# Fused attention and two gated layers on one core: x loaded by head sides, upper parts of W_out on ScalarE, layer-2 operand sums on GpSimd

## What is computed

```python
# attention: batch 4, 8 heads, 576 tokens, head size 64, block-causal mask
scores = scale * q @ k.T ; softmax ; attn @ v
# x: (2304 tokens, 512), heads side by side
h = x @ w_in                     # 512 -> 2048
g = h * clip(h + 3, 0, 6) / 6
x2 = g @ w_out                   # 2048 -> 512
h = x2 @ w2_in
g = h * tanh(softplus(h))
out = g @ w2_out
```

## Time and profile before

| What | Value |
|---|---|
| median of 3 runs | 977.72 us (974.49 to 978.66) |
| the profiled execution's own time | 975.95 us |
| its span | 974.0 us |
| PE busy | 952.0 us, 98% of the span |
| DVE, ACT, POOL busy | 746.6, 643.6, 431.3 us |
| mean granted clock of PE | 0.998 |

### The profile page before, as it was taken

The page is one execution under the profiler, slowest core; times in us unless marked ns, Lnnn a source line. Parts: engine busy times, 40 slices in busy tenths (PEclk is TensorE's granted clock), DMA queues, the critical chain, the costliest instruction groups (busy, mean ns, idle before and its releaser), DMA issues.

```text
span 974.0 us, 17754 instructions
## 1 busy us (share of the span) xinstructions
PE 952.0 (98%) x6028; PEld 848.0 (87%) x6028; DVE 746.6 (77%) x1417; ACT 643.6 (66%) x1431; POOL 431.3 (44%) x410
## 2 busy tenths in 40 slices
PE   8999999999999999999899999999999999999998
PEld 7898888999887888888788988998998988988896
DVE  7898898774868686789788787777887777777654
ACT  7999999754544445454445557777777777776663
POOL 7899779665837596776867670000000000000000
PEclk9999999999999999999999999999999999999999
DMA  7988898657698978788786546555655654565255
GB/s 217 270 240 243 258 273 234 173 153 238 220 291 291 290 256 252 234 294 252 269 275 212 209 170 217 176 202 195 215 197 184 231 210 155 182 248 187 90 193 194
DMA packets 84601, 216.42 MB, mean 222 GB/s; under 512 B 10144, under 2 KB 16928, under 8 KB 84512
## 3 DMA queue, kind: packets, MB, share of 16 engines
q1 hardware_dynamic: 84368, 215.01, 67.6%
q10 hardware_dynamic: 144, 0.29, 0.1%
HBM read 162.07 MB, written 39.92 MB: 207 GB/s over the span
## 4 chain that ended last, share of the span: by engine, by line
PE 67%; DVE 7%; DMA 6%; SPq 4%; POOL 3%; issue 2%; ACT 1%; ACTq 0%; DVEq 0%; POOLq 0%
PE psum L1021 32%; PE psum L904 10%; PE psum L906 10%; PE psum L905 10%; DMA ext_d<-ext_made 3%; PE psum L849 2%; PE psum L828 2%; DVE ebuf L1624 1%; PE psum L808 1%; POOL osplit L1885 1%; SPq L646 1%; DVE glo L1630 1%; PE psum L809 1%; SPq L648 1%; DVE ext_made L1530 1%
## 5 line engine op out<-in xcount | busy, mean ns | idle before, releaser
L1021 PE MATMUL psum<-ghi,osplit 128*128 128x512 f32 (+1 forms) x640 | 216.7, 372 | 2.1 <-POOL osplit L1885 2.1
L904 PE MATMUL psum<-xhi,whi 128*128 128x256 f32 (+1 forms) x640 | 188.0, 294 | 5.1 <-ACT snap L1242 2.5
L906 PE MATMUL psum<-xhi,wlo 128*128 128x256 f32 (+1 forms) x640 | 187.2, 293 | 0.0
L905 PE MATMUL psum<-xlo,whi 128*128 128x256 f32 (+1 forms) x640 | 187.0, 292 | 0.0
L1021 PE MATMUL psum<-osplit,ghi 128*128 128x512 f32 x576 | 180.7, 395 | 1.3 <-DVE glo L1630 1.3
L1630 DVE SCALAR_TENSOR_TENSOR glo<-ebuf,ghi 128x512 fp32r<-128x512 f32 x144 | 126.5, 878 | 22.9 <-ACT ghi L1290 14.8
L904 PEld LDWEIGHTS psum<-xhi,whi 128*128 128x128 f32 x640 | 121.1, 189 | 19.0 <-ACT snap L1242 4.4
L1290 ACT ACTIVATE ghi<-ebuf 128x512 fp32r<-128x512 f32 x144 | 90.4, 628 | 66.9 <-DVE ebuf L1624 46.2
L1021 PEld LDWEIGHTS psum<-ghi,osplit 128*128 128x128 f32 x640 | 118.5, 190 | 18.4 <-issue 2.7
L1885 POOL TENSOR_TENSOR osplit<-oraw,osplit 128x512 fp32r<-128x512 f32 x80 | 117.2, 1468 | 38.1 <-ACT osplit L1209 34.0
L905 PEld LDWEIGHTS psum<-xlo,whi 128*128 128x128 f32 x640 | 121.2, 189 | 10.5
(11 more groups left out here) (120 smaller groups left out, 2147.4 us busy)
## 6 DMA issues: line engine op xcount, KB each, us to landing
ext<-ext_d SPq DMA_DIRECT2D x56, 768.0 KB, 4.4
osplit<-o_d SPq DMA_DIRECT2D x80, 512.0 KB, 5.3
oraw<-in_w_out SPq DMA_DIRECT2D x80, 256.0 KB, 5.8
wraw<-in_w_in SPq DMA_DIRECT2D x26, 512.0 KB, 6.0
ext_d<-ext_made SPq DMA_DIRECT2D x32, 384.0 KB, 6.2
attn_t<-ostage SPq DMA_DIRECT2D x32, 288.0 KB, 3.7
qkin<-in_qk SPq DMA_DIRECT2D x30, 288.0 KB, 3.7
kparts<-kparts SPq DMA_DIRECT2D x30, 288.0 KB, 4.2
```

Source lines behind the costliest of these rows:

```text
L904: pe.matmul(dst, hi, xh, start=(start and cc == 0), stop=False, skip_group_check=True)
L905: pe.matmul(dst, hi, xl, start=False, stop=False, skip_group_check=True)
L906: last = pe.matmul(dst, lo, xh, start=False, stop=(stop and cc == 1), skip_group_check=True)
L1021: last = pe.matmul(bank(Y_BANK + c, n), stat, mov, start=(first and m == 0), stop=(final and m == 2), skip_group_check=True)
```

## The change

1. The x load of blocks 1 to 4 is made by sides in place of chunks (`load_x_side`): for side h two DMAs of the heads' summands (L656 of the new kernel) and one that spreads two rows of inverse sums (L660), so 6 DMAs for a half in place of 8, with the same bytes. For blocks 2 to 4 side 0 is issued near the head of SP's step, ahead of `load_ext`, and side 1 where the whole load stood.
2. W_out's hi parts of tiles 32 to 79 go from POOL to ACT (`first_os`, bound SPLIT_OS in place of ACT_OS).
3. The three sums for each pair of the second layer's extra operands go from DVE (`mix_w`) to POOL (`mix_late`), with a semaphore of their own, `late_mixed`.
4. On POOL in step 0 the sums of block 1's second half (`mix_x(1, 1)`) come one W_out tile later.

```diff
--- before.py
+++ after.py
@@ -118,7 +118,6 @@
 TILES = [(layer_of(g), t) for g in range(STEPS) for t in tiles_of(g)]
 TILE0 = [sum(len(tiles_of(k)) for k in range(g)) for g in range(STEPS + 1)]
 FIRST_OS = OR
-ACT_OS = TILE0[FIRST_STEP[2]]
 SPLIT_OS = TILE0[LAYER]
...
@@ -173,8 +172,8 @@
 X_SPLITS = per_block((3, 6, 8))
 X_MIXES = per_block((1, 2, 8))
 X_LOADS = [[sum(16 * n(b) for b in range(blk)) for blk in range(NBLK + 1)] for n in (
-    lambda b: (16 if KIND[b] == SHORT else 8) if b < NBL else 1,
-    lambda b: 0 if KIND[b] == SHORT else 8 if b < NBL else 2 if b > NBL else 1)]
+    lambda b: (16 if KIND[b] == SHORT else 6) if b < NBL else 1,
+    lambda b: 0 if KIND[b] == SHORT else 6 if b < NBL else 2 if b > NBL else 1)]

 JOBS = ([(0, p, True, False) for p in range(PAIRS)] + [(0, p, False, True) for p in range(PAIRS)] +
...
@@ -185,7 +184,7 @@
 NEARLY, HALVED = len(EARLY_JOBS), 6
 EARLY_LOADS = {0: (0, 0), 1: (0, 1), 2: (1, 0), 3: (1, 1), 6: (2, 0), 7: (2, 1), 9: (3, 0), 10: (3, 1),
                19: (4, 0), 20: (4, 1), 21: (5, 0), 22: (5, 1)}
-EARLY_X_LOAD, NEXT_X_LOAD = tuple(range(11, 19)), (27, 28, 29, 30)
+EARLY_X_LOAD, NEXT_X_LOAD = tuple(range(11, 19)), (27, 29)
 EARLY_X_ADD, EARLY_X_MIX = (19, 20, 21, 22), 23
 EARLY_X_HI, EARLY_X_LO = (23, 24, 25), (24, 25, 26)
 EARLY_O_LOAD = (23, 24, 25)
...
@@ -226,7 +225,8 @@

-MIXED = [sum(3 if e else 1 for _, _, _, e in JOBS[NEARLY:m]) for m in range(len(JOBS) + 1)]
+MIXED = [sum(0 if layer == 1 and e else 3 if e else 1 for layer, _, _, e in JOBS[NEARLY:m])
+         for m in range(len(JOBS) + 1)]

 def own(m):
...
@@ -649,7 +650,17 @@
                                  r_d[2 * c + h:2 * c + h + 1, cols].to_broadcast([DH, cols.stop - cols.start])
                                  ).then_inc(done, 16)
-            def load_x(blk, cc):
+            def load_x_side(x, cc, h, cols, done):
+                rows = slice(h * DH, (h + 1) * DH)
+                for i in range(2):
+                    sp.dma_start(x[rows, i, 0:2, :],
+                                 attn_t[4 * i + 2 * cc + h, :, cols].rearrange("(s d) t -> d s t", s=2)
+                                 ).then_inc(done, 16)
+                rinvs = r_d[2 * cc + h:HEADS:4, cols]
+                sp.dma_start(x[rows, :, 2, :], rinvs.unsqueeze(0).broadcast_to([DH, 2, cols.stop - cols.start])
+                             ).then_inc(done, 16)
+
+            def load_x(blk, cc, sides=range(2)):
                 t0 = first_token(blk)
                 cols = slice(t0, t0 + width(blk))
                 if blk >= LATE_X:
...
@@ -658,8 +669,8 @@
                     sp.wait_ge(x_lo, x_index(blk, cc, 0))
                 if blk < NBL:
                     attention_stored(-(-cols.stop // SEQ))
-                    for i in range(2):
-                        load_x_chunk(x_staged(blk, cc, i), 2 * i + cc, cols, x_loaded[cc])
+                    for h in sides:
+                        load_x_side(xst_late if blk == 1 and cc == 1 else xst, cc, h, cols, x_loaded[cc])
                     return
                 covered = sum(1 for b in range(NBL) if first_token(b) < cols.stop)
                 for c in range(DC):
...
@@ -676,14 +687,17 @@
                     for i in range(2):
                         sp.dma_start(x_staged(blk, 1, i)[:, 0, :], rows[1, :, i, :]).then_inc(x_loaded[1], 16)
-            def next_x(s):
+            def next_x(s, side):
                 for blk in range(2, LATE_X):
                     t = s - (FIRST_STEP[blk] - 2)
-                    if t == -8:
-                        load_x(blk, 0)
-                    if t == -4 and KIND[blk] == QUAD:
-                        load_x(blk, 1)
+                    sides = (side,) if blk < NBL else range(2 * side)
+                    if t == -8 and sides:
+                        load_x(blk, 0, sides)
+                    if t == -4 and sides and KIND[blk] == QUAD:
+                        load_x(blk, 1, sides)
+                if side == 0:
+                    return
                 for blk, t in late_blocks(s):
                     if t in LATE_LOAD and (LATE_LOAD[t] == 0 or KIND[blk] == QUAD):
                         load_x(blk, LATE_LOAD[t])
...
@@ -729,11 +743,10 @@
                 if n in EARLY_O_LOAD:
                     load_o(EARLY_O_LOAD.index(n))
                 if n in NEXT_X_LOAD:
-                    i, side = divmod(NEXT_X_LOAD.index(n), 2)
-                    if i == 0 and side == 0:
+                    if n == NEXT_X_LOAD[0]:
                         sp.wait_ge(x_lo, X_SPLITS[1])
                         attention_stored(2)
-                    load_x_chunk(x_staged(1, 0, i), 2 * i, slice(HT, HT + TB), x_loaded[0], (side,))
+                    load_x_side(xst, 0, NEXT_X_LOAD.index(n), slice(HT, HT + TB), x_loaded[0])
                 if in_use(n) and n != LAST:
                     store_o(n)
                 if in_use(n) and n != LAST and n % HEADS == HEADS - 1:
...
@@ -752,6 +765,7 @@
                         store_ext_hi(m)
                 for t in ahead_at(s - 1):
                     store_ahead_hi(t)
+                next_x(s, 0)
                 if quad(s + 3):
                     load_ext(s + 3)
                 if first_of_block(s):
...
@@ -776,7 +790,7 @@
                     stream_o(i)
                 for i in raw_at(s)[1:2]:
                     load_o(i)
-                next_x(s)
+                next_x(s, 1)
                 for i in raw_at(s)[2:]:
                     load_o(i)
                 for i in streams[2:]:
...
@@ -1157,7 +1171,10 @@
             def split_ext_hi(m):
                 layer, p, _, _ = JOBS[m]
-                act.wait_ge(w_mixed, MIXED[m + 1])
+                if layer == 0:
+                    act.wait_ge(w_mixed, MIXED[m + 1])
+                else:
+                    act.wait_ge(late_mixed, 3 * (p + 1))
                 act.wait_ge(ext_hi_stored, 16 * (layer * PAIRS + p))
                 nc.scalar.activation(ext_made[:, 0:EXT], wraw[m % 2][:, A_COLS:RES], ACT.Copy).then_inc(w_hi, 1)
...
@@ -1313,7 +1330,7 @@
             def first_os(s, k):
-                todo = [i for i in splits_at(s) if i < ACT_OS]
+                todo = [i for i in splits_at(s) if i < SPLIT_OS]
                 for i in todo[k:k + 1]:
                     split_o_hi(i)
...
@@ -1532,7 +1549,8 @@
             def mixing_jobs(s):
                 for m in jobs_at(s)[0:1]:
-                    mix_w(m)
+                    if JOBS[m][0] == 0 or JOBS[m][2]:
+                        mix_w(m)
             def resident_jobs(s):
                 for k, m in enumerate(jobs_at(s)):
...
@@ -1816,6 +1834,17 @@
                     add_x(1, 2)
                     scale_x(1, 2)
+            def mix_late(m):
+
+                p, raw = JOBS[m][1], wraw[m % 2]
+                a11, a12, a22, a21 = (raw[:, k * A_COLS:(k + 1) * A_COLS] for k in range(4))
+                pool.wait_ge(w_loaded[m % 2], w_level(m))
+                nc.gpsimd.tensor_tensor(a21, a11, a21, ALU.subtract).then_inc(late_mixed, 1)
+                pool.wait_ge(late_mixed, 3 * p + 1)
+                nc.gpsimd.tensor_tensor(a22, a22, a21, ALU.subtract).then_inc(late_mixed, 1)
+                pool.wait_ge(late_mixed, 3 * p + 2)
+                nc.gpsimd.tensor_tensor(a12, a12, a22, ALU.subtract).then_inc(late_mixed, 1)
+
             def split_early_hi(m):
                 pool.wait_ge(early_mixed, m + 1)
...
@@ -1874,12 +1903,12 @@
             def split_o(i):
                 o, raw = osplit[i % OS2], oraw[i % OR]
-                if i < FIRST_OS or i >= ACT_OS:
+                if i < FIRST_OS:
                     pool.wait_ge(o_loaded[i % OR], 16 * (i // OR + 1))
                     if i >= OS2:
                         pool.wait_ge(y_step, y_tile(i - OS2))
                     nc.gpsimd.tensor_copy(o[:, 0:D], raw[:, :]).then_inc(o_hi, 1)
-                    pool.wait_ge(o_hi, i + 1 if i < FIRST_OS else i + 1 - (ACT_OS - FIRST_OS))
+                    pool.wait_ge(o_hi, i + 1)
                 else:
                     pool.wait_ge(first_o_hi, i + 1 - FIRST_OS)
                 nc.gpsimd.tensor_tensor(o[:, D:2 * D], raw[:, :], o[:, 0:D].bitcast(F32), ALU.subtract
...
@@ -1925,10 +1954,14 @@
                 if s == 0:
                     add_x(1, 3)
                     scale_x(1, 3)
-                    mix_x(1, 1)
+                for m in jobs_at(s):
+                    if JOBS[m][0] == 1 and JOBS[m][3]:
+                        mix_late(m)
                 next_x(s, 0)
                 for i in todo[1:2]:
                     split_o(i)
+                if s == 0:
+                    mix_x(1, 1)
                 next_x(s, 1)
                 for i in todo[2:]:
                     split_o(i)
```

More of the change, by code:

```diff
@@ L368, in build @@
         w_mixed = sem("w_mixed")
+        late_mixed = sem("late_mixed")
         w_hi = sem("w_hi")
```

## The result

The change is slower. Nine runs of each kernel gave 982.80 us (978.05 to 986.65) against 976.68 us (974.12 to 979.12): a ratio of 1.0064, with a 95% interval of 1.0046 to 1.0082. The forecast was 971.6 us, in a range of 967.0 to 976.5. The profiled execution has a span of 981.6 us, against 974.0 before.

A forecast was written before the change was run, and what follows sets the result against it. It took PE's idle waits and a half-clock stretch, at most 11.7 us, as recoverable. Gains of 2.9 + 1.0 + 0.3 + 1.9 = 6.1 us took 975.95 to 969.85, plus 1.77 for the runs' median: 971.6 us, range 967.0 to 976.5.

The forecast's parts named there:

- the lo store's: Steps 19 to 26: the extra operands' lo store lands some 2 us earlier, so 0.5 us of PE's 2.32 us wait stay.
- steps 19 to 26: 425 to 500 us: sums moved to POOL remove 5.4 us of PE's waits, 3.5 are spent again, 1.9 us gained.
- the five short waits: PE's waits from 425 to 500 us other than the 2.32 us one: 3.1 us, from DVE's sums, all to go.
- Steps 0 and 1: Near 213 us: mix_x(1, 1) later on POOL ends PE's 2.10 us wait and half clock, 0.9 stay: 2.9 us gained.
- Blocks 2 and 3: Hi parts on ACT end the 402 us wait, 1.0 us; x by sides eases the 317 us wait, 0.3 us.
- The 0.3 us of the lo store's chain: PE's 1.46 us wait at 317 us, ending DVE's chain behind a lo store: 0.3 us gained, ends -1 and 1.46.
- Step 26: POOL's work on block 4's second x half ends late, so PE waits 2.5 us at step 26; ends 0 and 5.
- The 27.5: POOL's time in us from x's landing to its last lo part, with five casts gone and six sums added.
- Rival 4: ACT stands behind W_out's loads, 2 us lost in each of nine steps: slower, 989.6 us; chance 0.08.
- Rival 3: The shared SBUF port gives DVE's time back: 974.5 us, or 976.2 with the clock falling; sign POOL sums over 1.2; chance 0.12.
- Rival 2: POOL sets block 4's start, PE waits 5 us at step 26: 974.1 us; sign x landing after 18 us; chance 0.16.
- The slower case: Slower by over 0.5%: given only to ACT standing behind W_out's loads, 989.6 us; chance 0.08.

The follow-up runs named there:

- side0_late_step22: The change with side 0 of the x load moved back behind the lo store and second W_out tile in step 22 alone: ratio 1.0023 to the kernel before.
- before_again: The kernel before, unchanged, profiled once more; no ratio is given, and its wait of PE for tile 4 was 1.00 us.
- six_dmas: hi_on_act_alone with the x load by sides in six DMAs, all at the old place: ratio 0.9978 to the kernel before.
- side0_late: The change with side 0 of each x load of blocks 2 to 4 back just ahead of side 1: ratio 0.9998 to the kernel before.
- hi_on_pool: The change with the hi parts of W_out's tiles 32 to 79 back on POOL: ratio 1.0127 to the kernel before.
- hi_on_act_alone: The kernel before with only the hi parts of W_out's tiles 32 to 79 moved to ACT: ratio 0.9971 to the kernel before.

## Why the prediction was wrong

- **The failed step** is the lo store's, in the part on steps 19 to 26. The text saw all of it: "The store one step before now stands behind side 0's three DMAs on SP's queue, as do `ext`, the weights and a W_out tile, and side 0 waits at the step's head for POOL's lo parts of the first half. DVE without its sums has room for that." It put no price on that wait. The runs put about 4 us on it (`side0_late_step22` against the change) and show why the room didn't help: the chain runs through the single buffer of the lo part, and a DVE that waits for a store has no use for room. The price could have been bounded from rows of before: POOL's lo parts of the first half ended at 446.55, and three sums a step at 0.8 to 1.19 us, less two casts of 0.91, in three steps make them 1.8 to 5.3 us later, while the early place asks for them 3.6 us earlier (446.46 against 450.08). That is an estimate of 1.9 to 5.4 us of waiting for SP; the trace has 4.2.
- **What the sums' move did win:** the five short waits (3.1 us) that were to go from 425 to 500 us went but for one of 0.40 us. The long ones took their place.
- **Steps 0 and 1, 2.9 us:** nothing that the runs show (0.9992 alone). The signs were there (under 1 us, clock at full), but for another reason: the wait for tile 4 didn't go. It is 0.89 us in the change and 1.00 in `before_again`, and ACT's hi part sets it, not `mix_x`. The size was read from one execution in which `mix_x` took 1 us longer, the wait was twice its usual length and the clock fell.
- **Blocks 2 and 3, 1.0 + 0.3 us:** right in direction, and the hi parts on ACT were worth more than forecast, 2.8 us (0.7 to 5.1). The 0.3 us of the lo store's chain didn't show: PE's wait there was 1.46 us in before, 1.63 in `before_again` and 1.85 in the change. The early side 0 took some 2 us back: in step 2 its DMAs go ahead of two W_out tiles, ACT waited 2.78, 2.37 and 1.21 us for tiles where before waited 2.33 and 0.29, and PE 1.97 at 251. All five kernels with side 0 early in step 2 have a wait of 1.6 to 2.0 us there; of those without, one has 1.16 (`six_dmas`) and the others 0.3 or none. The prediction had "the bytes queued are the same", which is true and says nothing about which of them is needed first.
- **Step 26, 2.5 us:** the wait was forecast at 2.5 and measured at 2.41, and 2.40 in `side0_late`. That the number agrees in the change is luck: POOL's chain from its first work on x took 31.6 us, not 27.5, and x landed 19.7 us after step 22's start (457.34 + 9.6 against 447.26 on ACT), not 17.1, but PE had been delayed as much by its other waits. The 27.5 is also a slip: 27.4 - 4.5 + 4.8 is 27.7.
- **The rivals.** Rival 4's mechanism isn't it: ACT waited once for `oraw` after 425 us, 3.24 us, and PE didn't wait for that; `hi_on_pool` is slower yet. Rival 3: POOL's sums took 0.75 to 1.08 us on the mean, under the 1.2 that was its sign; DVE's lo parts of g were as long as before (1.17 us against 1.18), and DVE's instructions from 425 to 500 us took 49.89 / 61 = 0.82 us on the mean as 65.80 / 80 = 0.82 before. The Trainium skill's rule in page "SBUF — State Buffer", section "Who interferes with whom" (a DVE instruction with two SBUF inputs contends with a GpSimd one that reads SBUF), made no extra loss that this mean shows. Rival 2 held in part: x landed later than its sign of 18 us, but PE's wait at step 26 was 2.41 us and not 5. The slower case should have been the one with SP's queue, and had no chance of its own.
- The Trainium skill, page "DMA: Bandwidth & Descriptors", section "Anatomy of one DMA — SWDGE (gpsimd) path", says that a semaphore wait of a DMA happens on the sequencer that issues it, not in the DMA engines. The trace agrees: SP's queue stood 4.2 us for side 0 alone, and the lo store behind it, ready from 448.15 us, went out at 454.56.

## What to carry to other kernels

A DMA that waits for a semaphore is a barrier for everything behind it in its issuing queue: before moving one earlier, list what is behind it and compare the moment when the queue arrives there with the moment when its condition comes true, on the slowest engine's timeline and after the other parts of the change. Two moves that cost nothing alone can meet in one wait, so ask of each pair whether one makes the other's condition late. And a term that rests on one wait of one execution needs a second profile, above all where a fall of the clock hangs on it.

## Unexpected in the hardware

- The clock doesn't fall after every wait of the same length: it stayed at 2.4 GHz after 2.32 us and after the 2.41 us at 470 us in `hi_on_act_alone`, and fell for a few us after 2.10, 1.97 and 2.41 us in the profiles shown above. At one and the same place the 1.97 us at 251 in the change were followed by 0.59 from 252 to 256 us, and the 1.98 us at 251 in `side0_late_step22` by 1.00 from 250 to 256. A wait of 2 us is worth 2 or nearly 4 us from one execution to the next.
- A lo store of 384 KB took 8.4 us from issue (454.56) to landing (462.97) behind six DMAs, and 10.9 (455.40 to 466.28) behind the whole x load in `side0_late`. Over the whole changed kernel the stores of this size took 6.3 us at the median. So what stands ahead of such a store moves its landing by several us, which counts where a single buffer waits for it.
